# Attention and FFN kernel on one core: per-head scores on half the array rows, local softmax shifted on VectorE, and ten weight slabs split in FFN block 0

## The reference

```python
def sm_attn(qq, kk, vv):
    s = scale * np.matmul(qq, kk.transpose(0, 1, 3, 2))
    s = s - np.max(s, axis=-1, keepdims=True)
    a = np.exp(s)
    a = a / (np.sum(a, axis=-1, keepdims=True) + 1e-09)
    return np.matmul(a, vv)
q_d = q.reshape(B, H, Sd, 4, D).mean(axis=3)          # k_d, v_d alike; Sd = 144
out_up = np.repeat(sm_attn(q_d, k_d, v_d), 4, axis=2)
mask = np.abs(pos[:, None] - pos[None, :]) < 4
out_local = softmax(where(mask, scale * q @ k.T, -1e9)) @ v
x = (out_up + out_local), heads side by side          # 2304 x 512

h = x @ w_in                                           # 512 -> 2048
g = h * np.tanh(softplus(h))
x = g @ w_out                                          # 2048 -> 512

logits = x @ w_gate + modality_bias[modality_id]       # 8 experts, one per token
out[mask] = gate_w[mask, None] * (relu(x[mask] @ w1[e]) @ w2[e])
```

## Time and profile before

| | us |
|---|---|
| median of 3 executions | 946.95 (946.82 to 948.1) |
| the profiled execution: its span | 947.0 |
| attention, up to the last `xT` (L908) | 219.4 |
| PE busy over the span | 871.4 (92%) |
| DVE busy | 510.1 (54%) |
| ACT busy | 429.1 (45%) |
| POOL busy | 231.5 (24%) |

### The profile page before, as it was taken

How to read it: one execution, slowest core, us unless ns; L and a number is a source line. 1 busy time by engine, 2 the same in 40 slices (tenths; PEclk the granted TensorE clock), 3 DMA queues, 4 the chain that set the end, 5 groups by cost and what they waited for, 6 DMA issues and landing times.

```text
span 947.0 us, 16050 instructions
## 1 busy us (share of the span) xinstructions
PE 871.4 (92%) x4845; PEld 734.7 (78%) x4846; DVE 510.1 (54%) x1023; ACT 429.1 (45%) x1186; POOL 231.5 (24%) x218
## 2 busy tenths in 40 slices
PE   4888888879999999999999999987799999999995
PEld 3666666668988988989989989975577777777773
DVE  6999999945756555555555555675741111111110
ACT  3777777754555445454454454452152222222121
POOL 2667666542230010010010001252311111111110
PEclk9899999969999999999999999998899999999997
DMA  5555555211100000000000000310331011110110
GB/s 117 149 147 149 148 148 147 56 43 45 45 1 34 1 1 33 0 0 33 0 0 33 0 0 34 115 64 34 127 107 45 22 44 44 43 39 28 44 44 12
DMA packets 88197, 51.57 MB, mean 54 GB/s; under 512 B 64480, under 2 KB 77280, under 8 KB 88160
## 3 DMA queue, kind: packets, MB, share of 16 engines
q1 hardware_dynamic: 85040, 41.16, 15.5%
q0 software_dynamic: 3120, 9.96, 3.1%
HBM read 41.67 MB, written 9.70 MB: 54 GB/s over the span
## 4 chain that ended last, share of the span: by engine, by line
PE 67%; DVE 14%; issue 6%; DMA 5%; ACT 3%; POOL 2%; DVEq 1%; SPq 0%; ACTq 0%; POOLq 0%
PE ps L1326 7%; PE ps L1327 7%; PE ps L1328 7%; PE ps L1302 6%; PE ps L1301 6%; PE ps L1307 6%; PE ps L1436 6%; PE ps L1438 6%; PE ps L1437 6%; DMA xg<-y_rows,gidx 4%; DVE smax L889 3%; DVE ssum L899 3%; DVE kdz L874 2%; DMA vwin<-in_v_dram 2%; PE ps L1227 1%
## 5 line engine op out<-in xcount | busy, mean ns | idle before, releaser
L988 DVE TENSOR_SCALAR Tb<-Eb 128x384 f32<-128x384 f32 x96 | 41.4, 431 | 133.9 <-ACT Eb L733 133.9
L733 ACT ACTIVATE Eb<-ps 128x384 f32<-128x384 f32 x96 | 47.1, 491 | 141.7 <-PE ps L1307 141.6
L1302 PE MATMUL ps<-xh,WA 128*128 128x384 f32 x288 | 98.3, 341 | 0.0
L663 ACT ACTIVATE prob<-ps,nmax 96x111 f32<-96x111 f32 (+1 forms) x256 | 87.8, 356 | 23.0 <-DVE nmax L893 22.7
L1301 PE MATMUL ps<-xh,WA 128*128 128x384 f32 x288 | 97.8, 340 | 0.0
L562 POOL TENSOR_TENSOR xl<-xT,xh 128x384 fp32r<-128x384 f32 x24 | 26.8, 1144 | 280.4 <-ACT xh L705 280.4
L1326 PE MATMUL ps<-WA,gh 128*128 128x512 f32 x216 | 87.1, 403 | 2.4 <-DVE gl L947 2.4
L1328 PE MATMUL ps<-WA,gl 128*128 128x512 f32 x216 | 85.4, 395 | 0.0
L1327 PE MATMUL ps<-WA,gh 128*128 128x512 f32 x216 | 85.2, 394 | 0.0
L1167 DVE TENSOR_TENSOR hTl<-ps,hTh 128x1024 fp32r<-128x1024 f32 x19 | 23.3, 1225 | 112.5 <-ACT hTh L796 112.5
L742 ACT ACTIVATE Rb<-Tb 128x384 f32<-128x384 f32 x96 | 50.5, 526 | 73.6 <-DVE Tb L990 73.6
(11 more groups left out here) (218 smaller groups left out, 2078.6 us busy)
## 6 DMA issues: line engine op xcount, KB each, us to landing
wsraw<-in_moe_w_dram SPq DMA_DIRECT2D x32, 256.0 KB, 3.2
vwin<-in_v_dram SPq DMA_DIRECT2D x32, 166.5 KB
qraw<-in_q_dram SPq DMA_DIRECT2D x32, 144.0 KB, 3.0
kraw<-in_k_dram SPq DMA_DIRECT2D x32, 144.0 KB, 3.1
vdraw<-in_v_dram SPq DMA_DIRECT2D x32, 144.0 KB
y_rows<-yrow SPq DMA_DIRECT2D x6, 768.0 KB, 3.6
wraw<-in_moe_w_in_dram SPq DMA_DIRECT2D x12, 256.0 KB, 5.6
wraw<-in_moe_w_out_dram SPq DMA_DIRECT2D x12, 256.0 KB, 3.5
```

The source lines that it names most:

```text
L663: last = act.activation(prob[0:np_, a.s6, n * w:(n + 1) * w], ps[0:np_, o:o + w], ACT.Exp, scale=sc, bias=nmax[0:np_, a.s6, n:n + 1], accu ...
L1302: pe.matmul(dst, lo, xh[:, kk, :], start=False, stop=False)
```

## The change

1. The window of keys is 105 wide, not 111. Windows 0 to 2 start at 0, 93, 186, windows 3 to 5 at 285, 378, 471 (`KBASE`), so `vwin` is loaded with four DMAs for an item, each of 105 partitions and three windows.
2. `kz` and `kdz` become `kT` and `kdT` without zeros. Scores are made for one head at a time, on the 64 partitions of that head, into one PSUM bank for each head. The mask is added for three tiles at once, 315 columns, twice per unit. The memsets at the start are gone, round 2 is copied by ACT, and each pooling of k is one instruction over 128 partitions.
3. In local units DVE adds the negative maximum to the scores on their way from PSUM to `prob` (`shift`), ACT takes one exponential over 630 columns in place, and DVE sums the six groups (`add_sums`). The pooled unit keeps its biases and four activations. PE's `scores` of a unit can begin when the unit two before it is shifted (for kind 2: when kind 0 has its exponentials).
4. `times_v` alternates between the two heads.
5. Slabs 0 to 5 are split in attention, one for every two items, and slabs 6 to 15 in FFN block 0, one at each of the steps 0 to 9, through two staging buffers. The first two of these loads are issued when the last `xT` is written; each later one waits for the low part of the slab two before it.

```diff
-    KSTEP, KW = 93, 111
+    KSTEP, KW = 93, 105
+    KBASE = [KSTEP * t if t < NHF else S - KW - KSTEP * (NT - 1 - t) for t in range(NT)]
...
-        kz = alloc(att, "kz", [P, 2, 2, S])
-        kdz = alloc(att, "kdz", [P, 2, 2, SD])
+        kT = alloc(att, "kT", [P, 2, S])
+        kdT = alloc(att, "kdT", [P, 2, SD])
-        wraw = alloc(att, "wraw", [P, 2, 2 * DM])
+        wraw = alloc(att, "wraw", [P, 2 * DM])
...
+        def slab_stage(j):
+            return ystage[:, (j % 2) * 2 * DM:(j % 2 + 1) * 2 * DM]
+        NPRE = NPAIR // 2 - 2
...
-                if is_k:
-                    copy(kz[0:D, a.par, 0, lo:hi], src[0:D])
-                    last = copy(kz[D:P, a.par, 1, lo:hi], src[D:P])
+                last = copy((kT if is_k else qT)[:, a.par, lo:hi], src)
...
-                    sp.dma_start(vwin[:, par, :, h, :], v_windows[head + b * H]).then_inc(v_in[par], 16)
+                    for hf in range(2):
+                        sp.dma_start(vwin[:, par, hf * NHF:(hf + 1) * NHF, h, :], v_windows[hf][head + b * H]
+                                     ).then_inc(v_in[par], 16)
...
+                if (n - V_LAG) % 2 == 0:
+                    j = hp * (B // 2) + (n - V_LAG) // 2
+                    if not static or j < NPRE:
+                        wait(sp, w_lo, j)
+                        load_slab(j, wraw, wraw_in)
...
-            for j in range(NWA, NF):
-                sp.wait_ge(w_lo, j)
+            for j in range(NPRE, NF):
+                wait(sp, w_lo, max(NPRE, j - 1))
+                load_slab(j, slab_stage(j), late_in[j % 2])
...
+                if a.kind != 0:
+                    pr = prob[0:QT, a.s6, :]
+                    act.activation(pr, pr, ACT.Exp, scale=SCALE).then_inc(exped, 1)
+                    return
...
-                if a and a.kind != DVE_ROUND:
+                if a:
                     copy_turned(act.copy, act, a, a.kind)
...
-                    if first_block and j % 3 == 2 and NWA + j // 3 < NF:
-                        late_slab_hi(NWA + j // 3)
+                    if first_block and NPRE + j < NF:
+                        late_slab_hi(NPRE + j)
...
-            dve.memset(kz[:, :, :, :], 0.0)
-            dve.memset(kdz[:, :, :, :], 0.0).then_inc(kz_clear, 1)
...
+                    dst, src = (kdT, kT) if is_k else (qdT, qT)
...
+                dve.tensor_tensor(
+                    prob[0:QT, a.s6, :].rearrange("p (h t w) -> p h t w", h=2, t=NHF), scores_ap(a),
+                    smax[0:QT, a.s6, 0:6].rearrange("p (h t) -> p h t", h=2).unsqueeze(3).to_broadcast([QT, 2, NHF, KW]),
+                    ALU.add).then_inc(biased, 1)
...
+                    dve.tensor_reduce(ssum[0:QT, a.s6, 0:6], prob[0:QT, a.s6, :].rearrange("p (n w) -> p n w", n=6),
+                                      AXX, ALU.add).then_inc(summed, 1)
...
+                b, c = At(m, dn, RECIP), At(m, dn, MAXIMA)
+                if b.on:
+                    add_sums(b)
+                if c.on:
+                    maxima(c)
+                if b.on:
+                    add_eps(b)
+                if c.on:
+                    shift(c)
+                if b.on:
+                    invert_sums(b)
...
-            copy_turned(dve.tensor_copy, dve, At(0, 0, 0), DVE_ROUND)
...
-                wait(pe, exped, a.u - 1)
+                wait(pe, exped if a.kind == 2 else biased, a.u - 1)
...
+                    for h in range(2):
+                        pe.matmul(ps[0:QT, o[h]:o[h] + NHF * KW], identb[0:QT, 0:QT],
+                                  mask[:, t0:t0 + NHF, :].rearrange("p t w -> p (t w)"), start=True, stop=False)
+                    for t in range(NHF):
+                        tt = t0 + t
+                        for h in range(2):
+                            last = pe.matmul(ps[0:QT, o[h] + t * KW:o[h] + (t + 1) * KW],
+                                             qT[h * D:(h + 1) * D, a.par, tt * QT:(tt + 1) * QT],
+                                             kT[h * D:(h + 1) * D, a.par, KBASE[tt]:KBASE[tt] + KW],
+                                             start=False, stop=(t == NHF - 1))
```

More of the change, by code:

```diff
@@ L351, in build @@
         vdv = v.rearrange("b h (c p r) d -> b h p c (r d)", c=2, r=FACT)
-        v_windows = bass.AP(tensor=v.tensor, offset=v.offset,
-                            ap=[[S * D, B * H], [D, KW], [KSTEP * D, NT], [1, D]])
+        v_windows = [bass.AP(tensor=v.tensor, offset=v.offset + KBASE[n * NHF] * D,
+                             ap=[[S * D, B * H], [D, KW], [KSTEP * D, NHF], [1, D]]) for n in range(2)]
         win_v = w_in.rearrange("(kk p) n -> p kk n", p=P)
@@ L514, in _ @@
             link(pool.memset(mask[:, :, :], 0.0))
[L515 to L518, removed]
+            for hf in range(2):
+                off = QT * hf * NHF - KBASE[hf * NHF]
+                part = mask[:, hf * NHF:(hf + 1) * NHF, :]
+                link(pool.affine_select(out=part, in_=part, compare_op=ALU.is_ge, fill=-1e30,
+                                        base=FACT - 1 + off, pattern=[[lead, NHF], [-1, KW]], channel_multiplier=1))
+                link(pool.affine_select(out=part, in_=part, compare_op=ALU.is_ge, fill=-1e30,
+                                        base=FACT - 1 - off, pattern=[[-lead, NHF], [1, KW]], channel_multiplier=-1))
             def sum_v(a):
-                pool.wait_ge(v_in[a.par], a.gen * 64 + 64)
+                pool.wait_ge(v_in[a.par], a.gen * 96 + 96)
                 wait(pool, pv, 3 * a.p - 5)
@@ L552, in step @@
                     sum_v(a)
-                if has_slab(m) and dn % 3 == 1:
-                    split_lo(m * 2 + (dn // 3 - SLAB_LAG), wraw[:, dn // 3], True)
+                if has_slab(m) and dn == 1:
+                    split_lo(m - 1, wraw, True)
             attention_steps(pool, step)
@@ L565, in _ @@
             x_part_lo(0)
-            for j in range(NWA, NF):
-                split_lo(j, yrow[:, 0:2, :].rearrange("p a b -> p (a b)"))
+            for j in range(NPRE, NF):
+                split_lo(j, slab_stage(j))
             with pool.Fori(1, NTB) as i:
@@ L696, in step @@
                 a = turned_item(m, dn, 0)
-                if a and a.kind != DVE_ROUND:
+                if a:
                     copy_turned(act.copy, act, a, a.kind)
-            for r in range(ROUNDS - 1):
+            for r in range(ROUNDS):
                 copy_turned(act.copy, act, At(0, 0, 0), r)
@@ new lines, in maxima, with shift @@
+            def maxima(a):
+                np_, n = (QD, 4) if a.kind == 0 else (QT, 6)
+                dve.wait_ge(scored, a.u + 1)
+                wait(dve, exped, a.u - 5)
+                dve.tensor_reduce(smax[0:np_, a.s6, 0:n].rearrange("p (h t) -> p h t", h=2), scores_ap(a), AXX,
+                                  ALU.max, negate=True).then_inc(maxed, 1)
+            def shift(a):
+                dve.wait_ge(maxed, a.u + 1)
+                if a.kind == 0:
+                    dve.tensor_scalar(nmax[0:QD, a.s6, 0:4], smax[0:QD, a.s6, 0:4], SCALE / (FACT * FACT), None,
+                                      ALU.mult).then_inc(biased, 1)
+                    return
+                wait(dve, probT, a.u - 5)
+                dve.tensor_tensor(
+                    prob[0:QT, a.s6, :].rearrange("p (h t w) -> p h t w", h=2, t=NHF), scores_ap(a),
+                    smax[0:QT, a.s6, 0:6].rearrange("p (h t) -> p h t", h=2).unsqueeze(3).to_broadcast([QT, 2, NHF, KW]),
+                    ALU.add).then_inc(biased, 1)
@@ L1212, in scores @@
             def scores(a):
-                wait(pe, exped, a.u - 1)
-                o = a.s2 * 2 * BANK
+                wait(pe, exped if a.kind == 2 else biased, a.u - 1)
+                o = [(a.s2 * 2 + h) * BANK for h in range(2)]
                 if a.kind == 0:
```

136 lines of the change are left out of this document (53 added, 83 removed).

## The result

| | before | after |
|---|---|---|
| median of 4 runs, us | 946.88 (946.5 to 948.1) | 986.44 (984.44 to 988.1) |
| ratio, 95% interval | | 1.042 (1.040 to 1.044) |
| profiled execution, span, us | 947.0 | 986.3 |

A forecast was written before the change was run, and what follows sets the result against it. Attention was taken as bound by the loop that loads v's windows (11.89 us per item), the FFN by PE. 947.0 - 1.5 (start) - 22.3 (pace) - 7.5 (end of attention) + 14.5 (FFN block 0) = 930.2 us; range 917 to 948.

The forecast's parts named there:

- B: Pace of attention: faster v load, DVE waiting less for POOL, item from 11.89 to 10.3 us: -22.3 us.
- D: FFN block 0: ten late slabs in a row make PE wait for `gl`: +14.5 us, bounds +3 and +17.
- Rival 4: Attention: PE becomes the bound through 64-row score matmuls, one more us per item, pace 11.2, 944 us; chance 0.11.
- A: Start of attention: round 2 of k takes one ACT copy and one DVE pooling, first maximum earlier: -1.5 us.
- C: End of attention: the last unit's `normalise` no longer waits for the last `sum_v`: -7.5 us, bounds -3.5 and -9.

The follow-up runs named there:

- the kernel with added work: Changed kernel plus two full-row matmuls of 512 columns ahead of each unit's scores: 922.3 us in one execution, 927.9 us when timed.
- the full-row kernel: Changed kernel with every score matmul on all 128 rows instead of one head's 64 (each score sums both heads): 928.1 us, executed once.

## Why the prediction was wrong

- **The step that failed** is in part B: "PE falls by little if halves of the array do not overlap and to about 8.5 if they do", put beside a pace of 10.3 that DVE was to set. The halves overlap, and at the upper clock level the work is 8.0 us, so the size was nearly right. But 10.0 and 8.5 hold only at the clock of the stretch that they were read from (granted 0.93), and I carried that clock over to the changed kernel without a reason; I had thought of a falling clock in D alone. In the changed kernel TensorE stayed at its lower level, was busy 200.00 us of 200, and set the pace itself: 14.11 us per item, +31.2 us where I had -22.3. What holds the level down is that the scores stand on half the rows, and not the time that the overlap saves: without overlap the level was low as well (17.5 us per item). Why half rows do this is open; the runs show only with which kernels it happens.
- **Rival 4** had the right engine and place, PE in its score matmuls, and a wrong reason and size: 1 us per item against 4.0 (14.11 - 10.09). The Trainium skill's page "TensorEngine Tiling", section "Key Properties", which I weighed there, says that a change of tiling mode drains TensorE. The traces agree in so far as they show a gap at such a place at full clock: between 60 and 140 us the weight loads of half-row scores stand idle 3.8 us ahead of 16 groups (0.24 each) in the kernel with added work, those of full-row scores 0.2 us in all. That is 0.5 us per item, and the kernel that has it keeps a pace of 10.03: it was not the cause.
- **The rest of B** was right. With half rows taken away and all else kept, the pace is 10.09 (forecast 10.3). `sum_v` waits 1.6 us in all; shift and sum take 0.81 and 0.79 (forecast 0.80); the small addition has a mean of 0.34 (0.54 on full rows, forecast under 0.6). The load of v was the pacer: windows of 105 in four loads gave -3.2%, though at 97 to 168 GB/s and not at over 200. The saving on the slabs did not come: their copies took 0.41 us each before the change, 24 of them, and take 0.85 in the changed kernel, 12 of them, so DVE is freed of nothing there and not of 0.4 us per item.
- **A**: first maximum at 13.10, -2.0 against -1.5 said. **C**: on full rows, from item 15 to the last `xT` 184.34 - 163.05 = 21.3 us against 29.3 before, -8.0 against -7.5. In the changed kernel itself, at the lower level, it is -2.5.
- **D** was right to half a microsecond at its place. After the change (issue by SP, PE's first, fourth and tenth `ffn_out`):

```profile
246.83 0.39 SPq L430 DMA_DIRECT2D ystage<-in_moe_w_in_dram  x1
```

```profile
255.09 0.80 PE L1355 MATMUL ps<-WA,gh 128*128 128x512 f32 x1 [4.43 <-DVE gl L968]
...
270.94 0.50 PE L1355 MATMUL ps<-WA,gh 128*128 128x512 f32 x1 [0.85 <-DVE gl L968]
...
302.74 0.50 PE L1355 MATMUL ps<-WA,gh 128*128 128x512 f32 x1 [0.89 <-DVE gl L968]
```

  302.74 - 246.83 = 55.9 us (forecast 56.1), against 261.15 - 219.38 = 41.8 before (forecast 41.6): +14.1. The steps are 5.30 apart (5.33). PE's waits are 0.85 and not 1.15, since its own step is 4.45 with them. Over the whole rest of the program only 11.9 of the 14.1 is seen; on the kernel with windows of 105 it is 16.6, on the full-row kernel 13.9. What makes these 2 us to and fro behind block 0 I did not trace.
- With the clock at its upper level the forecast of 930 would have been near: the full-row kernel took 928.1 us, and its parts lie near the terms of the sum (first maxima -1.4, pace -25.2, end of attention -8.0, rest +13.9 us). It is a kernel with other work on PE, executed once; the changed kernel with the added work took 922.3 and 927.9 us.

## What to carry to other kernels

A busy PE at "1.00" may be a PE at half speed: compare the duration of a group that the change did not touch with the same group at a known clock, before any theory on what keeps PE busy. And ask of each saving on TensorE whether what is left keeps the clock up; where DVE or DMA sets the pace, matmuls that are padded with zeros can be worth more than the work they waste. Look at the partition count of a slow DMA first: the windows of 105 in four loads were worth 3%, all the rest of this change together less than nothing.

## What was not expected of the hardware

- In these profiles the column of the granted clock shows 1.00 until the first time that it falls, even at the lower level: here for the whole of attention, 246 us at 1.2 GHz by the durations (384 columns in 0.32 us).
- The Trainium skill's page "TensorE: Matmul & The Clock Gate", section "Part 1: The HAM clock gate (the "warmup" mystery)", says that the throttled state is the default and activity releases it. The trace agrees: in the kernel before, `turn`'s four matmuls take 0.90 us at 8.59 and 0.52 at 19.82. The changed kernel adds that an engine without any idle time can stay throttled: 200.00 us busy of the 200 from 40 to 240.
- Both levels can hold on the same instructions: some 50 us at 0.50 and then 1.00 up to 180 us, with one added matmul of 512 columns per unit (one execution).
- Two 64-row matmuls for different heads and banks do run side by side: a unit's twelve take 1.30 us in place of 2.34 at the lower clock.
